# Fused attention and two feed-forward layers on Trainium2: the first product's inputs split by other engines, the centroid chain moved behind the second w3 tile

## What is computed

```python
q_n, k_n, c_n = (x / (norm(x) + 1e-06) for x in (q, k, centroids))
q_assign = argmax(q_n @ c_n.T); k_assign = argmax(k_n @ c_n.T)
scores = where(q_assign[:, None] == k_assign[None, :], scale * q @ k.T, -1e9)
attn_out = softmax(scores) @ v
x = attn_out with the heads side by side
x = ((x @ w1) * (x @ w2)) @ w3 @ w_out
h = x @ w_in
out = (max(h, 0) + alpha * min(h, 0)) @ w_out2
```

## Time and profile before

| | us |
|---|---|
| median of three runs | 748.01 |
| the profiled execution | 747.64 |
| its span, first to last instruction | 745.8 |
| TensorE matmul, busy | 739.0 (99%) |
| VectorE, busy | 411.8 (55%) |
| ScalarE, busy | 311.6 (42%) |
| GpSimd, busy | 179.5 (24%) |

### The profile page before, as it was taken

One profiled execution on the slowest core, in us unless ns is written; L12 is line 12 of the kernel. 1 busy time (PEld: TensorE's weight loads), 2 busy tenths in 40 slices (PEclk: granted clock), 3 DMA queues, 4 the chain that ended last, 5 costly groups with the idle time before them and its releaser, 6 DMA issues.

```text
span 745.8 us, 10690 instructions
## 1 busy us (share of the span) xinstructions
PE 739.0 (99%) x3792; PEld 641.6 (86%) x3792; DVE 411.8 (55%) x632; ACT 311.6 (42%) x623; POOL 179.5 (24%) x211
## 2 busy tenths in 40 slices
PE   8999999999999999999999999999999999999998
PEld 6888999999999998888888888888888888888886
DVE  4435999999999984721311432575434333343432
ACT  5235988988988884311211422432012111121111
POOL 2141566866865893500000000000000000000000
PEclk9999999999999999999999999999999999999999
DMA  9636366566566233300000022140001000010001
GB/s 293 195 94 144 78 152 155 124 146 154 127 146 153 65 84 92 98 29 1 1 0 1 20 93 85 57 130 11 1 0 57 1 0 1 1 56 1 1 0 57
DMA packets 65371, 54.17 MB, mean 73 GB/s; under 512 B 32032, under 2 KB 54576, under 8 KB 65328
## 3 DMA queue, kind: packets, MB, share of 16 engines
q1 hardware_dynamic: 65328, 53.59, 27.9%
HBM read 31.50 MB, written 3.19 MB: 47 GB/s over the span
## 4 chain that ended last, share of the span: by engine, by line
PE 97%; DVE 1%; DMA 1%; ACT 1%; issue 0%; SPq 0%; DVEq 0%; ACTq 0%
PE slot L625 63%; PE acc L625 24%; PE slot L689 9%; PE acc L638 1%; PE slot L737 1%; DMA early<-in_moe_w_out 1%; DVE xl L1163 0%; DVE xl L1145 0%; ACT xh L938 0%; ACT xh L945 0%; DVE abx L1283 0%; DVE ab L1279 0%; ACT abx L1055 0%; ACT asb L1041 0%; ACT ost L1108 0%
## 5 line engine op out<-in xcount | busy, mean ns | idle before, releaser
L625 PE MATMUL slot<-xh,w 128*128 128x512 f32 x768 | 248.0, 389 | 0.0
L625 PEld LDWEIGHTS slot<-xh,w 128*128 128x128 f32 x768 | 144.1, 188 | 29.8
L625 PE MATMUL slot<-xl,w 128*128 128x512 f32 x384 | 149.4, 389 | 0.0
L1101 ACT CAST gh<-gf 128x512 fp32r<-128x512 f32 x48 | 29.9, 623 | 203.2 <-PE acc L625 186.0
L1206 DVE TENSOR_TENSOR pl<-slot,ph 128x384 fp32r<-128x384 f32 x192 | 97.6, 549 | 8.5 <-ACT ph L973 8.2
L1200 DVE TENSOR_REDUCE nm<-slot 128x1 f32<-128x768 f32 x96 | 91.4, 952 | 15.4 <-PE slot L625 13.8
L973 ACT CAST ph<-slot 128x384 fp32r<-128x384 f32 x192 | 83.5, 489 | 34.3 <-PE slot L689 33.8
L965 ACT ACTIVATE pf<-slot,nm 128x768 f32<-128x768 f32 x96 | 88.4, 921 | 4.6 <-DVE nm L1200 4.5
L625 PEld LDWEIGHTS slot<-xl,w 128*128 128x128 f32 x384 | 72.1, 188 | 15.0
L625 PE MATMUL slot<-k,q 80*128 80x384 f32 (+1 forms) x384 | 82.9, 337 | 0.0
L1329 DVE TENSOR_TENSOR gl<-gf,gh 128x512 fp32r<-128x512 f32 x48 | 33.2, 692 | 89.9 <-ACT gh L1101 89.9
(11 more groups left out here) (121 smaller groups left out, 1012.0 us busy)
## 6 DMA issues: line engine op xcount, KB each, us to landing
stage<-in_moe_w SPq DMA_DIRECT2D x16, 256.0 KB, 3.5
stage<-in_moe_w_in SPq DMA_DIRECT2D x16, 256.0 KB, 2.7
stage<-in_moe_w_out SPq DMA_DIRECT2D x16, 256.0 KB, 3.0
stage<-in_moe_w SPq DMA_DIRECT2D x6, 512.0 KB, 4.2
qk<-in_q SPq DMA_DIRECT2D x16, 192.0 KB, 3.9
qk<-in_k SPq DMA_DIRECT2D x16, 192.0 KB, 3.9
vn<-in_v SPq DMA_DIRECT2D x16, 192.0 KB, 3.8
q<-k SPq DMA_DIRECT2D x16, 192.0 KB, 3.8
```

The source lines that it names most:

```text
L625: return nc.tensor.matmul(o, a, b, start=start, stop=stop)
L1101: copy(gh[j % 2][:, :], gf[j % 2][:, :]).then_inc(gh_done, 1)
```

## The change

It moves the centroid chain, loads included, behind the second w3 tile on SyncE, ScalarE, VectorE and TensorE. w_out's first quarter is cast by VectorE and subtracted by GpSimd, under semaphores of their own, so ScalarE begins with w3 tile 0; the counts of piece_hi and piece_lo are one lower from there on. GpSimd writes the zeros ahead of the identity. TensorE's first product is taken in the order in which its parts come: high x high and low x high of a quarter, then high x low. The second set of spins is 4 and not 6. The transposes of cn and alpha come between the halves of the second product, and head 0's transposes of q and k behind both halves.

```diff
--- before.py
+++ after.py
@@ -208,6 +208,7 @@
         setup_pool, setup_act = sem("setup_pool"), sem("setup_act")
         cen_turned, table_done = sem("cen_turned"), sem("table_done")
         piece_hi, piece_lo = sem("piece_hi"), sem("piece_lo")
+        wo_first_hi, wo_first_lo = sem("wo_first_hi"), sem("wo_first_lo")
         front_hi, front_lo = sem("front_hi"), sem("front_lo")
         w3_turned, w3_hi, w3_lo = sem("w3_turned"), sem("w3_hi"), sem("w3_lo")
         wc_full, wc_out = sem("wc_full"), sem("wc_out")
@@ -237,9 +238,9 @@
         W34_EARLY = NF + 1
         X_FREE, FOLD_FREE = 2, 1
         NWO = NF // 2
-        READY_W12, READY_W34 = NWO - W12_EARLY, NWO - W12_EARLY + NF
+        READY_W12, READY_W34 = NWO - 1 - W12_EARLY, NWO - 1 - W12_EARLY + NF
         W3_STAGED = 3
-        IDENT, ZEROS, OPERANDS = 2, 3, 5
+        ZEROS, IDENT, OPERANDS = 1, 3, 5
 
         def staged(e, piece):
 
@@ -381,13 +382,12 @@
                 if c % T6 == 4 and (not last or c // T6 + 2 < HB):
                     next_v(it, c // T6 + 2)
 
-            sp.dma_start(cn[:, :], cen.rearrange("h c d -> (h c) d")).then_inc(ld_cen, 16)
             load_w3(0, 0)
-            load_wo(0)
-            sp.dma_start(al16, alpha.rearrange("(j p) -> j p", p=P)).then_inc(ld_al, 16)
-            for i in range(1, NWO):
+            for i in range(NWO):
                 load_wo(i)
             load_w3(1, 1)
+            sp.dma_start(cn[:, :], cen.rearrange("h c d -> (h c) d")).then_inc(ld_cen, 16)
+            sp.dma_start(al16, alpha.rearrange("(j p) -> j p", p=P)).then_inc(ld_al, 16)
             for f in (2, 3):
                 sp.dma_start(early[NWO + f - 2][:, :], w3d[f]).then_inc(ld_early[NWO + f - 2], 16)
             load_qk(0, 0)
@@ -453,10 +453,10 @@
                 ins.then_inc(setup_pool, 1)
                 pool.wait_ge(setup_pool, count[0])
 
+            ordered(nc.gpsimd.memset(cwin[0][:, :].bitcast(F32), 0.0))
             ordered(nc.gpsimd.memset(ident[:, :], 0.0))
             ordered(nc.gpsimd.affine_select(out=ident[:, :], in_=ident[:, :], compare_op=ALU.not_equal, fill=1.0,
                                             base=0, pattern=[[-1, P]], channel_multiplier=1))
-            ordered(nc.gpsimd.memset(cwin[0][:, :].bitcast(F32), 0.0))
             ordered(nc.gpsimd.memset(scl[:, :], 1.0))
             ordered(nc.gpsimd.memset(scl[0:D, :], SCALE))
             ordered(nc.gpsimd.memset(zero[:, :], 0.0))
@@ -584,6 +584,10 @@
                 if u == 4 and out_head % 2:
                     x_lo(it, out_head)
 
+            pool.wait_ge(wo_first_hi, 1)
+            nc.gpsimd.tensor_tensor(wol[:, 0:2, :], early[0][:, :].rearrange("p (a n) -> p a n", a=2),
+                                    woh[:, 0:2, :].bitcast(F32), ALU.subtract).then_inc(wo_first_lo, 1)
+            pool.wait_ge(wo_first_lo, 1)
             pool.wait_ge(table_done, 2)
             for j in range(HB):
                 window(0, j)
@@ -747,19 +751,19 @@
                 if g == NF - 1:
                     last.then_inc(wc_full, 1)
 
-            def product_first():
-
-                o = slot[0][:, 0, :]
-                pe.wait_ge(piece_hi, 1)
-                pe.wait_ge(w3_hi, 1)
-                for g in range(2):
-                    mm(o, w3h[:, 0, g, :], woh[:, g, :], g == 0, False)
-                pe.wait_ge(piece_lo, 1)
-                for g in range(2):
-                    mm(o, w3h[:, 0, g, :], wol[:, g, :], False, False)
-                pe.wait_ge(w3_lo, 1)
-                for g in range(2):
-                    mm(o, w3l[:, 0, g, :], woh[:, g, :], False, False)
+            def first_high(i):
+                for g in (2 * i, 2 * i + 1):
+                    mm(slot[0][:, 0, :], w3h[:, 0, g, :], woh[:, g, :], g == 0, False)
+
+            def first_low(i):
+                for g in (2 * i, 2 * i + 1):
+                    mm(slot[0][:, 0, :], w3l[:, 0, g, :], woh[:, g, :], False, False)
+
+            def first_cross(i):
+                for g in (2 * i, 2 * i + 1):
+                    last = mm(slot[0][:, 0, :], w3h[:, 0, g, :], wol[:, g, :], False, g == NF - 1)
+                if i == NWO - 1:
+                    last.then_inc(wc_full, 1)
 
             def product_tile(f, parity):
                 pe.wait_ge(w3_lo, f + 1)
@@ -773,27 +777,36 @@
 
             pe.wait_ge(setup_pool, ZEROS)
             spin(8)
+            pe.wait_ge(setup_pool, IDENT)
             turn_w3(0, 0)
+            spin(4)
+            pe.wait_ge(wo_first_hi, 1)
+            pe.wait_ge(w3_hi, 1)
+            first_high(0)
+            pe.wait_ge(w3_lo, 1)
+            first_low(0)
+            for i in range(1, NWO):
+                if i == NWO - 1:
+                    turn_w3(1, 1)
+                pe.wait_ge(piece_hi, i)
+                first_high(i)
+                first_low(i)
+                if i == 1:
+                    pe.wait_ge(wo_first_lo, 1)
+                    first_cross(0)
+                pe.wait_ge(piece_lo, i)
+                first_cross(i)
+            turn_w3(2, 0)
+            pe.wait_ge(w3_lo, 2)
+            product_wc(1, range(NF // 2))
             pe.wait_ge(setup_act, 1)
             nc.tensor.transpose(acc[0:D, 0, 0:P], cn[:, :], ident[:, :])
             pe.wait_ge(ld_al, 16)
             nc.tensor.transpose(acc[:, 1, 0:NJ], al16, ident[0:NJ, 0:NJ]).then_inc(cen_turned, 1)
-            spin(6)
-            product_first()
-            pe.wait_ge(piece_lo, 2)
-            product_wc(0, (2, 3))
-            pe.wait_ge(piece_lo, 3)
-            product_wc(0, (4, 5))
-            turn_w3(1, 1)
-            pe.wait_ge(piece_lo, NWO)
-            product_wc(0, (6, 7))
-            turn_w3(2, 0)
-            pe.wait_ge(w3_lo, 2)
-            product_wc(1, range(NF // 2))
+            product_wc(1, range(NF // 2, NF))
             pe.wait_ge(table_done, 2)
             for half in range(2):
                 turned(0, 0, half, True)
-            product_wc(1, range(NF // 2, NF))
             for f in range(2, NF - 2):
                 turn_w3(f + 1, (f + 1) % 2)
                 for half in range(2):
@@ -925,13 +938,14 @@
         def _(act):
             copy = nc.scalar.copy
 
-            act.wait_ge(ld_cen, 16)
-            nc.scalar.activation(xf[0][:, 0, 0:D], cn[:, :], ACT.Square, accum_out=cs[:, 0:1]).then_inc(act_step, 1)
-            act.wait_ge(dve_step, 1)
-            nc.scalar.activation(cs[:, 2:3], cs[:, 1:2], ACT.Sqrt).then_inc(act_step, 1)
-            act.wait_ge(dve_step, CEN_DVE)
-            nc.scalar.mul(cn[:, :], cn[:, :], cs[:, 3:4]).then_inc(setup_act, 1)
-
+            def centroids():
+
+                act.wait_ge(ld_cen, 16)
+                nc.scalar.activation(xf[0][:, 0, 0:D], cn[:, :], ACT.Square, accum_out=cs[:, 0:1]).then_inc(act_step, 1)
+                act.wait_ge(dve_step, 1)
+                nc.scalar.activation(cs[:, 2:3], cs[:, 1:2], ACT.Sqrt).then_inc(act_step, 1)
+                act.wait_ge(dve_step, CEN_DVE)
+                nc.scalar.mul(cn[:, :], cn[:, :], cs[:, 3:4]).then_inc(setup_act, 1)
 
             def wo_hi(i):
                 act.wait_ge(ld_early[i], 16)
@@ -995,12 +1009,12 @@
                     probabilities(it, c)
 
             act.wait_ge(setup_pool, OPERANDS)
-            wo_hi(0)
             w3_hi_part(0, 0)
             wo_hi(1)
             wo_hi(2)
             wo_hi(3)
             w3_hi_part(1, 1)
+            centroids()
             w3_hi_part(2, 0)
             wc_copy(0, 0)
             for half in range(2):
@@ -1130,20 +1144,22 @@
                 dve.wait_ge(dve_step, count[0])
 
 
-            dve.wait_ge(act_step, 1)
-            ordered(nc.vector.tensor_scalar_max(cs[:, 1:2], cs[:, 0:1], 2.0 ** -100))
-            dve.wait_ge(act_step, 2)
-            ordered(nc.vector.reciprocal(cs[:, 3:4], cs[:, 2:3]))
-            ordered(tt_(cs[:, 3:4], cs[:, 3:4], cs[:, 0:1], ALU.mult))
-            ordered(tt_(cs[:, 3:4], cs[:, 3:4], cs[:, 2:3], ALU.add))
-            ordered(ts(cs[:, 3:4], cs[:, 3:4], 0.5, 1e-6, ALU.mult, ALU.add))
-            ordered(nc.vector.reciprocal(cs[:, 3:4], cs[:, 3:4]))
-            assert count[0] == CEN_DVE
-
             def wo_lo(i):
-                dve.wait_ge(piece_hi, i + 1)
+                dve.wait_ge(piece_hi, i)
                 tt_(wol[:, 2 * i:2 * i + 2, :], early[i][:, :].rearrange("p (a n) -> p a n", a=2),
                     f32(woh[:, 2 * i:2 * i + 2, :]), ALU.subtract).then_inc(piece_lo, 1)
+
+            def centroid_scales():
+
+                dve.wait_ge(act_step, 1)
+                ordered(nc.vector.tensor_scalar_max(cs[:, 1:2], cs[:, 0:1], 2.0 ** -100))
+                dve.wait_ge(act_step, 2)
+                ordered(nc.vector.reciprocal(cs[:, 3:4], cs[:, 2:3]))
+                ordered(tt_(cs[:, 3:4], cs[:, 3:4], cs[:, 0:1], ALU.mult))
+                ordered(tt_(cs[:, 3:4], cs[:, 3:4], cs[:, 2:3], ALU.add))
+                ordered(ts(cs[:, 3:4], cs[:, 3:4], 0.5, 1e-6, ALU.mult, ALU.add))
```

(6 more changed lines are left out.)

## The result

The changed kernel takes 749.76 us, the median of 14 runs, against 747.93 for the kernel before in the same rounds: a ratio of 1.0023, 95% interval 1.0016 to 1.0030. Forecast was a gain of 0.4 us; measured is a loss of 1.8. Its 14 runs also lie far apart, from 747.99 to 750.84, where those of the kernel before lie within 0.7 us: five at 748.0 to 748.6 with a mean granted clock of 0.999, three near 749.7 at 0.998, six at 750.5 to 750.8 at 0.997 to 0.998. The profiled one is of the last group: 750.6, span 748.8.

A forecast was written before the change was run, and what follows sets the result against it. TensorE, busy 99% of the span, bounds the kernel, so only its waits can be gained. Sum: 1.75 - 0.46 - 0.3 - 0.6 = 0.4 us gained, 747.6 by the median; range 746.4 to 749.0.

The forecast's parts named there:

- one load for Square: ScalarE, behind its cast of the second w3 tile: a table load from 14.34 to 15.62, then 3.29 us to scaled centroids.
- The front: Opening up to the second w3 tile's product: it starts at 15.63 in place of 17.38, 1.75 us earlier.
- rival (1): Table loads or waits off the path, first load ahead of everything: gain 1.3 to 1.5 or 2.0, 746.0 to 746.7; 12%.
- rival 4: TensorE's clock in the opening: 2.4 GHz level comes only at 11 or so, 1.4 to 2.7 later, 749.0 to 750.3; 7%.
- VectorE's copy: High part of wo's first quarter on VectorE: 1.2 us taken, 5.95 to 7.15, covered by ScalarE's cast.
- GpSimd's subtraction: Low part of wo's first quarter on GpSimd: 2.39 us, 7.2 to 9.6, there before TensorE needs it, covered.
- Wait for the scaled centroids: Middle of the second product: TensorE waits from 18.5 to 18.96 for ScalarE's scaled centroids, 0.46 lost.
- Transposes: The two of centroids and alpha, between the second product's halves: 0.3 lost with the refill, bounds 0.2 to 0.7.
- Head 0: Its q and k transposes, now behind the second product: TensorE waits for VectorE's splits, 0.6 lost, 0.3 if ScalarE is quick.
- (3): ScalarE's chain longer, in mid second product: loads costing twice their row add 2.57 us, 750.2; 6%.
- (2): Opening transfers do not move: second quarter at 8.44, second tile at 12.33, front gains 1.3, total 748.1; 15%.
- the wait on k: Sign in the changed profile: TensorE waits on VectorE's k near 23.

The follow-up runs named there:

- e2: Changed kernel with 12 spins in place of 4 before the first product, the table load left where it was: 748.80 us.
- e1: Changed kernel with a one-element Square added on ScalarE before its wait for the first w3 tile, bringing the table load early: 747.45 us, ratio 0.9994.
- e7: Changed kernel with the table load early (one-element Square) and 0 spins in place of 4 before the first product: 748.78 us.
- e4: Changed kernel with the centroid chain back at the front, head 0's transposes back between the halves and six spins; quarter split kept: 747.14 us, ratio 0.9989.
- e10: Kernel before with the centroid chain alone moved, plus a one-element Square ahead of wo's first-quarter cast: 748.35 us, ratio 1.0007.
- e6: Changed kernel with the table load early and head 1's q and k transposes moved into the middle of the third product: 746.97 us, ratio 0.9990.
- e5: Kernel before with the centroid chain alone moved behind the second w3 tile, wo's first quarter left with ScalarE and VectorE: 749.09 us, ratio 1.0018.
- e8: Changed kernel with the centroid chain woven into the front behind the first w3 tile, six spins, head 0 back between the halves: 751.72 us.
- e9: Centroid chain woven into the front behind the first w3 tile, with GpSimd's subtraction also held until VectorE's chain steps are done: 749.24 us.

## Why the prediction was wrong

**The step that failed** is in the part behind the second tile: "ScalarE's casts show none ahead of them. So I count one load for Square (14.34 to 15.62)". The front has ScalarE's first cast at 6.25 and no load ahead of it, so that a load there stands in the sum at nothing. The casts of before showed none because the chain had loaded tables ahead of them. The first instruction of ScalarE brings one in every trace here; it went to the first w3 cast, behind the cast's wait, and cost the path 1.38 us (e2 less e1). I had seen that the load "stood at the head of the stream", and took it only for a reason to hope, in rival (1). The rest of the loss is the clock that fell behind the pause: 1.50 in the profiled run, a term that the sum has at nothing too (rival 4).

**Term by term**, by e1, which is the change without that load and with a steady clock. Front: second product at 15.88, 1.50 earlier; I had 1.75. VectorE's copy took 0.69, under both my bounds (0.93 and 1.22), and was covered as said. GpSimd's subtraction took 2.38 and was covered. Wait for the scaled centroids: I had 0.46, there was none, as the Square's load was gone (cn was scaled at 17.76, TensorE came to it at 18.90). Transposes: I had 0.3; 0.27 in the chain, and the half behind them takes 2.95 where it took 2.75, 0.47 together. Head 0: I had 0.6; from 22.12 to 24.91 are 2.79 where 0.65 + 0.87 + 0.66 = 2.18 would do, 0.61. Sum: 1.50 - 0.47 - 0.61 = 0.42 against the 0.44 seen and the 0.4 forecast. That it meets the forecast is luck in part: the front was 0.25 short, and a wait of 0.46 that did not come made up for it. And I took the time behind the opening as unchanged: e1 loses 0.25 of its 0.44 there, and the changed kernel 0.5. A later stretch that gives the time back was one of the signs of my being wrong.

**The rivals.** (4), the clock, came true in most runs of the changed kernel, and I gave it 7%. Its price was right (1.4 to 2.7; measured 1.50 in the profiled run, 2.2 between the outer groups), its cause was not, in the profiled run: not a level that rises late, but one that was up at 8.74 (two matmuls in 0.70) and falls again behind TensorE's wait for the cast. For e7's slowest runs the late rise is not ruled out. Front error and clock are one chain of causes: the load makes the pause, the pause the low level. (3) named the right engine's loads, at the wrong place; it said 2.57 for two loads that cost double. The drain that the Trainium skill adds (ScalarE: Activation LUTs, section "What ACT_TABLE_LOAD costs") is in no trace here: the Sqrt of e4 starts 0.01 behind its load too. (2) did not come true: w3's first tile was turned at 4.26, VectorE had the first quarter at 5.48, 0.9 before the 6.40 of before, and e1's ScalarE the second at 8.03 where it was 8.42; but e1's chain, over a transfer until 8.01, and e10's, until 9.92, show that the landings bind next. (1) asked for the load at the head of the stream; e1 puts it there and gives 747.45, not 746.0 to 746.7, because head 0's wait remained; e6 takes that away and gives 746.97, still above, with 0.6 of the 1.0 that it had gained at the third product's end lost later. One reading of rows 5 was wrong as well: the 1.96 us that I took for VectorE's pace beside GpSimd is a mean over four, 1.23 to 2.87 (below).

**The signs** I had named: the w3 casts came at 7.58 and 16.42 in place of 6.3 and 13.3; one table load, not two, stood behind the second; no wait on cn, which I had named as a sign of my being wrong; the wait on k was there; the third product came at 27.79, past the 26.9 from which I would be wrong; and a later stretch did not give time back but took 0.5 more.

## What to carry to other kernels

Before moving the first work of an engine, ask what else its first instruction does: here a table load went with whatever came first, behind that instruction's wait. Give an engine with tables one trivial instruction with no operand to wait for at its start. And where the matmul engine has to wait a microsecond early on, keep it at work, since the price of the pause is paid by the work behind it, and only in some runs: compare the spread of runs, not the median alone.

## What the hardware showed that I had not expected

ScalarE's plain casts, too, want a table: the load of 1.28 us stands ahead of whichever instruction is its first (Square, cast, or the one-element Square of e1), and was issued ahead of it at once where the program has one wait there (0.74 in the kernel before, 0.73 in e1), and only behind the second wait where it has two (6.29 in the changed kernel, 5.32 in e5).

TensorE's granted clock fell to the 1.2 GHz level behind a stretch in which it was busy 0.70 of 2.00 us (changed kernel, 7 to 9 us). With the stretch filled by spins (e2) it stayed at 2.4 GHz in the profile and no run took over 749.2. In e8 it fell behind 2.55 us without a matmul, in all five runs. Which runs fall is not explained here: the same program gives both.

VectorE waits for GpSimd when both read two SBUF operands: VectorE's instruction ends only behind GpSimd's whole one (2.22 us for one element per partition in e8), while VectorE's subtraction with one operand in PSUM ran beside it at its usual 1.23 us (e1, 7.07 to 8.30, with GpSimd from 6.80 to 9.18). The 1.96 us of the earlier trace rows is a mean of such waits and not a slower rate: in the kernel before the four subtractions took 1.23, 2.87, 2.53 and 1.23, and the two long ones ended at 302.61 and 310.02, each 1.08 or 1.09 behind the GpSimd instruction that was under way when they began. The Trainium skill, GPSIMD Engine Reference, section "8. Key points", has contention of the two for SBUF interfaces with two SBUF inputs of VectorE; the traces agree, and put its size here at the rest of the GpSimd instruction (10.26 against 10.24 in e8, 11.80 + 1.08 = 12.88 in e9).
